# Chunk loads between the moves of x, ScalarE's output copies around a rounding, VectorE's extra work at the head of a slot

## What is computed

```python
w = np.exp(weight - np.max(weight, axis=-1, keepdims=True))
w = w / (np.sum(w, axis=-1, keepdims=True) + 1e-09)
x = np.einsum('hk,bskhg->bshg', w, x_unf)       # x_unf: each token and the 6 before it
h = x @ w_in                                     # first MLP
g = np.where(h >= 1, h, np.where(h <= -1, 0.0, (h + 1) ** 2 / 4))
x = g @ w_out
h = x @ w_in2                                    # second MLP
out = (h * (1.0 / (1.0 + np.exp(-1.702 * h)))) @ w_out2
```

## Time and profile before

| | |
|---|---|
| median of 3 runs | 1178.54 us (1177.29 to 1178.9) |
| the profiled execution | 1179.53 us |
| its span, first to last instruction | 1177.8 us |
| busy, share of the span | PE 97%, weight load 87%, DVE 70%, ACT 68%, POOL 36% |
| mean granted clock of PE | 0.993 of full speed |

### The profile page before, as it was taken

How to read it: one execution, slowest core, us unless ns; L and a number is a source line. 1 busy time by engine, 2 the same in 40 slices (tenths; PEclk the granted TensorE clock), 3 DMA queues, 4 the chain that set the end, 5 groups by cost and what they waited for, 6 DMA issues and landing times.

```text
span 1177.8 us, 25920 instructions
## 1 busy us (share of the span) xinstructions
PE 1146.4 (97%) x9382; PEld 1021.9 (87%) x9382; DVE 820.4 (70%) x1206; ACT 795.8 (68%) x1510; POOL 429.1 (36%) x425
## 2 busy tenths in 40 slices
PE   7999889999999999999999999999999999999998
PEld 4768679989989999889988999888988988899987
DVE  6877557677676867767677686767767676676633
ACT  4866476776867677686776767677676766765554
POOL 5892909053170714508062260804408062000000
PEclk9999989999999999999999999999999999999999
DMA  6312010001010010100001010010101000000001
GB/s 192 97 40 71 2 35 15 35 3 47 1 48 1 10 40 1 48 1 15 35 5 44 1 48 2 12 37 1 48 1 48 1 7 9 2 15 3 14 1 28
DMA packets 63857, 31.27 MB, mean 27 GB/s; under 512 B 56084, under 2 KB 60562, under 8 KB 63760
## 3 DMA queue, kind: packets, MB, share of 16 engines
q1 hardware_dynamic: 63760, 29.80, 9.5%
HBM read 23.09 MB, written 6.29 MB: 25 GB/s over the span
## 4 chain that ended last, share of the span: by engine, by line
PE 71%; ACT 11%; issue 6%; DVE 6%; POOL 5%; DVEq 0%; ACTq 0%; POOLq 0%
ACT raw L986 3%; ACT clip L936 3%; DVE gate L1103 3%; PE acc_all L748 3%; PE acc_all L762 2%; PE acc_all L754 2%; PE acc_all L757 2%; PE acc_all L759 2%; PE acc_all L765 2%; PE h_all L697 2%; PE h_all L699 2%; PE h_all L701 2%; PE h_all L692 2%; PE h_all L695 2%; PE acc_all L738 2%
## 5 line engine op out<-in xcount | busy, mean ns | idle before, releaser
L1109 DVE TENSOR_TENSOR g_lo<-gate,g_hi 128x512 fp32r<-128x512 f32 x232 | 190.0, 819 | 153.0 <-ACT g_hi L942 153.0
L942 ACT ACTIVATE g_hi<-gate 128x512 fp32r<-128x512 f32 x232 | 146.5, 632 | 201.0 <-DVE gate L1103 199.4
L1115 DVE TENSOR_TENSOR g_lo<-h_all,g_hi 128x512 fp32r<-128x512 f32 x256 | 175.0, 684 | 117.7 <-ACT h_all L953 115.8
L950 ACT ACTIVATE g_hi<-h_all 128x512 fp32r<-128x512 f32 x256 | 152.9, 597 | 87.1 <-PE h_all L703 58.1
L508 POOL TENSOR_TENSOR x_conv<-x_in,tap_w 128x384 f32<-128x384 f32 (+1 forms) x29 | 24.8, 875 | 508.8 <-ACT raw L986 506.5
L936 ACT ACTIVATE clip<-clip,half 128x512 f32<-128x512 f32 x256 | 184.3, 720 | 34.8 <-DVE clip L1094 32.6
L1094 DVE TENSOR_SCALAR clip<-h_all 128x512 f32<-128x512 f32 x256 | 174.8, 683 | 23.5 <-PE h_all L701 19.9
L508 POOL TENSOR_TENSOR prod<-x_in,tap_w 128x384 f32<-128x384 f32 (+1 forms) x174 | 181.2, 1065 | 4.2
L515 POOL TENSOR_TENSOR x_conv<-x_conv,prod 128x384 f32<-128x384 f32 (+1 forms) x174 | 179.8, 1055 | 1.6
L1103 DVE TENSOR_TENSOR gate<-h_all,clip 128x512 f32<-128x512 f32 x232 | 159.3, 687 | 19.5 <-ACT clip L936 8.7
L953 ACT ACTIVATE h_all<-h_all 128x512 f32<-128x512 f32 x256 | 151.6, 592 | 0.1
(11 more groups left out here) (281 smaller groups left out, 4766.0 us busy)
## 6 DMA issues: line engine op xcount, KB each, us to landing
x_in<-in_x SPq DMA_DIRECT2D x14, 960.0 KB, 4.8
out_y<-raw SPq DMA_DIRECT2D x360, 16.0 KB, 1.4
raw<-in_moe_w_out SPq DMA_DIRECT2D x6, 384.0 KB, 4.0
raw<-in_moe_w_in SPq DMA_DIRECT2D x4, 512.0 KB, 3.8
raw<-in_moe_w_in SPq DMA_DIRECT2D x8, 256.0 KB, 4.5
stage<-in_moe_w_out SPq DMA_DIRECT2D x2, 384.0 KB, 7.5
x_in<-in_x SPq DMA_DIRECT2D x1, 768.0 KB, 11.0
x_in<-in_x SPq DMA_DIRECT2D x2, 283.5 KB
```

The lines of the kernel that those rows point to most:

```text
L942: nc.scalar.activation(g1_hi[step.s % G_RING][:, :], gate1_of(step)[:, :], ACT.Copy).then_inc(g1_hi_ready, 1)
L950: nc.scalar.activation(g2_hi[step.s % G_RING][:, :], src, ACT.Gelu_apprx_sigmoid).then_inc(g2_hi_ready, 1)
L1109: nc.vector.tensor_tensor(g1_lo[k][:, :], gate1_of(step)[:, :], g1_hi[k][:, :].bitcast(FP32), ALU.subtract).then_inc(g1_lo_ready, 1)
L1115: nc.vector.tensor_tensor(g2_lo[k][:, :], bank2(step)[:, :], g2_hi[k][:, :].bitcast(FP32), ALU.subtract).then_inc(g2_lo_ready, 1)
```

## The change

The edit has four parts.

1. SP issues the moves of groups 0 to 2 (twelve transfers), then the loads of chunks 14 and 15, then the moves of groups 3 to 5. ACT rounds chunk 14 in slot 27 and chunk 15 in slot 28, not both in slot 31.
2. For tile 2's x the two parts are apart: transposes in slots 29 and 30 (both in 29 before), roundings in 29 and 30 (both in 29), low parts in 30 and 31 (both in 30).
3. ACT's copy of the main output sum stands ahead of the rounding of slot 8's gate, the copy of the rest behind it.
4. On DVE the additional work (transposes of x and of outputs, low parts of x, the last part of y) stands at the head of a slot, ahead of residue1, one slot later than before; the last part of y stays in slot 2.

```diff
-        EARLY = dict(move={3: [0], 4: [1], 5: [2], 6: [3], 7: [4], 9: [5]}, turn={7: [0], 10: [1]},
-                     hi={10: [0], 11: [1]}, lo={11: [0], 12: [1]})
-
-        LATE = dict(move={}, turn={13: [0, 1]}, hi={13: [0, 1]}, lo={14: [0, 1]})
+        EARLY = dict(move={3: [0], 4: [1], 5: [2], 6: [3], 7: [4], 9: [5]}, turn={8: [0], 11: [1]},
+                     hi={10: [0], 11: [1]}, lo={12: [0], 13: [1]})
+
+        LATE = dict(move={}, turn={13: [0], 14: [1]}, hi={13: [0], 14: [1]}, lo={14: [0], 15: [1]})
...
-            move_x()
+            sp.wait_ge(conv_step, 2 * CONV_STEPS)
+
+            sp.wait_ge(wp_ready, RAW_ORDER[0][-1] + 1 - DVE_CHUNKS)
+            move_x(range(MOVES // 2))
+
             for n in range(14, 2 * N_CHUNKS):
                 load_raw(n)
+            move_x(range(MOVES // 2, MOVES))
...
-                           24: [(13, 0)], 25: [(13, 1)], 31: [(14, 0), (14, 1), (15, 0), (15, 1)]}
+                           24: [(13, 0)], 25: [(13, 1)], 27: [(14, 0), (14, 1)], 28: [(15, 0), (15, 1)]}
...
+                if takes_out(tile) and s == OUT_SLOT:
+                    take_out(tile - 2, 0)
                 if one is not None:
                     round_gate1(one)
...
                 if takes_out(tile) and s == OUT_SLOT:
-                    take_out(tile - 2)
+                    take_out(tile - 2, 1)
...
                 solo = is_solo(tile, s)
+                at_y = s - shift_y(tile)
+                if takes_y(tile) and not solo and at_y == 2:
+                    take_y(tile - 1, 1 - side, 2)
+
+                if takes_out(tile) and s == OUT_SLOT + 6:
+                    turn_main(tile - 2)
+                if takes_out(tile) and s == OUT_SLOT + 7:
+                    turn_rest(tile - 2)
+                if prepares(tile):
+                    at = prep(tile)
+                    for part in at["turn"].get(s, ()):
+                        turn_x(tile + 1, part)
+                    for part in at["lo"].get(s, ()):
+                        split_x(tile + 1, 1 - side, part)
```

More of the change, by code:

```diff
@@ L431, in _, with move_x @@
             load(3)
-            def move_x():
-                sp.wait_ge(conv_step, 2 * CONV_STEPS)
-                sp.wait_ge(wp_ready, RAW_ORDER[0][-1] + 1 - DVE_CHUNKS)
-                for group in range(MOVES):
+            def move_x(groups):
+                for group in groups:
                     main = group < DM // BLOCK
@@ L965, in take_y, with take_out @@
                     nc.scalar.activation(rest[0:DR, :], y_part[0:DR, :], ACT.Copy).then_inc(y_from_act, 1)
-            def take_out(tile):
+            def take_out(tile, part):
                 main, rest = acc2
-                act.wait_ge(down2_done, (tile + 1) * F_TILES)
-                nc.scalar.activation(out_main, main[:, :], ACT.Copy).then_inc(out_copied, 1)
-                nc.scalar.activation(out_rest, rest[DR:P, :], ACT.Copy).then_inc(out_copied, 1)
+                if part == 0:
+                    act.wait_ge(down2_done, (tile + 1) * F_TILES)
+                    nc.scalar.activation(out_main, main[:, :], ACT.Copy).then_inc(out_copied, 1)
+                else:
+                    nc.scalar.activation(out_rest, rest[DR:P, :], ACT.Copy).then_inc(out_copied, 1)
             def take_x(tile, banks):
@@ L1202, in slot @@
                     residue1(before1)
-                at_y = s - shift_y(tile)
-                if takes_y(tile) and (at_y == 2 or solo and at_y == 1):
+                if takes_y(tile) and solo and at_y in (1, 2):
                     take_y(tile - 1, 1 - side, at_y)
-                if takes_out(tile) and s == OUT_SLOT + 5:
-                    turn_main(tile - 2)
-                if takes_out(tile) and s == OUT_SLOT + 6:
-                    turn_rest(tile - 2)
-                if prepares(tile):
-                    at = prep(tile)
-                    for part in at["turn"].get(s, ()):
-                        turn_x(tile + 1, part)
-                    for part in at["lo"].get(s, ()):
-                        split_x(tile + 1, 1 - side, part)
                 if two is not None:
```

## The result

The changed kernel takes **1175.97 us** (median, 1173.06 to 1176.88), beside 1178.78 us (1177.29 to 1179.02) for the kernel before on the same chip: a ratio of 0.9973, 95% interval 0.996 to 0.9986. It is faster, but by 0.3% where 1.0% was forecast, and it lies above the range. Its profiled execution took 1176.4 us, with a span of 1174.6 us.

The account below looks back on a forecast made before the run. PE, busy for 97% of the span, was taken as the bound, so only its standstills counted. 13.4 + 4.1 + 1.2 - 5.6 - 0.5 - 0.5 = 12.1 us gained, median 1178.54 to 1166.4 us; range 1159.5 to 1172.5.

Parts of the forecast that it names:

- the last part of y: Head of DVE's slot 2: PE loses 0.40 us in slot 3, 14 times, 5.6 us; 0.5 more in tile 2.
- the low parts of tile 2's x: Head of DVE's slots 30 and 31: wait for ACT's rounding delays g_lo once each, set at nothing, up to 0.8 us.
- the transposes of x: Head of DVE's slots 8 and 11: inputs ready slots before, so they cost next to nothing.
- The hole: PE's slots 37 and 38: ACT's wait for POOL, PE's standstill and the slow clock go, gaining 13.4 us.
- the queue of SP: Chunk loads between SP's moves: last twelve moves run from 98.8 to 106.8, last block in place at 108.6.
- the start of the convolution: POOL's convolution starts at 108.7, ends at 134.7; ACT comes to its move at 136.85, 2.1 us to spare.
- The wait for chunk 14: ACT's slot 27: the gate's rounding comes 1.7 us late; PE feels 0 to 1.0 us of it, taken as 0.5.
- Rival 4: Slots 12, 13: low parts of x meet POOL's additions, 1.0 us per tile, 13 us in all: 1180.6; chance 0.08.
- The port: DVE instructions with two SBUF inputs and POOL's exclude each other; trace agreed, price left to the fourth rival.
- The output copies: Slot 10 of a tile: main copy fits ahead of ACT's rounding, 0.34 us back 12 times, gaining 4.1 us.
- Slot 14: Slot 14 loses 0.20 us in twelve tiles; moving DVE's mid-slot work to the head regains half, 1.2 us.

Follow-up runs that it names:

- y_mid: Changed kernel with the last part of y again in the middle of DVE's slot 2, behind the clip: 1164.6 us, ratio 0.987.
- thin_add: Changed kernel with POOL's additions for tiles 3 to 15 cut to 8 columns, output not the reference's: 1171.75 us, ratio 0.9943.
- x_round_first: Changed kernel, y's last part and later tiles' low parts of x back mid-slot, ACT's roundings of tile 2's x ahead of the gate's: 1162.09 us.
- out_alone: Kernel before with only the two output copies on both sides of the rounding: 1173.25 us, ratio 0.9945.
- y_head_alone: Kernel before with only the last part of y moved to the head of DVE's slot 2: 1188.39 us, ratio 1.0098.
- turn_mid: Changed kernel with DVE's transposes of x for tiles 3 and later back in the middle of the slot before: 1173.03 us, ratio 0.995.
- thin_conv: Changed kernel with POOL convolving only the first of 8 heads for tiles 3 to 15, output not the reference's: 1168.08 us, ratio 0.9909.
- y_copy_first: Changed kernel with ACT's third copy of y ahead of the rounding of the gate in slot 1: 1165.16 us, ratio 0.989.
- short_pool: Changed kernel with POOL's convolution of tiles 4 to 15 in twice as many instructions of half the length: 1171.83 us, ratio 0.9939.
- short_best: x_round_first with POOL's convolution instructions of tiles 4 to 15 at half length: 1164.89 us, ratio 0.9883.

## Why the prediction was wrong

**What failed.** The profiled execution gained 9.0 us less than forecast (3.1 for 12.1). The step that failed is the price of the head of DVE's slot, which was too low. Its three wrong terms are the last part of y (priced at 0.40 us in each tile, measured 0.69, in tile 2 1.84 for the 0.9), the low parts of tile 2's x ("at nothing", measured 1.95 in slot 31), and the transposes of x ("costs next to nothing", 3.1 us in slot 12). Together they make 9.7 us. Slot 34 (slot 2 of tile 2), slot 13 and slot 14 add 1.8 us, and slot 10, chunk 14 and all others give 2.5 back.

**The hole, the queue of SP, the start of the convolution**: right, to a few tenths of a microsecond. The convolution itself ended at 136.08 and not at 134.7: it took 27.4 us, where 26.0 was called the most. ACT would have come at 136.85 by the forecast, so the room was 0.8 us and not 2.1; it was enough, and ACT came only at 140.68, since the slots before had grown.

**The last part of y** was the right mechanism with the wrong size; this is the largest miss (8.9 us against 5.2 in tiles 3 to 15, and in tile 2 slot 35 takes 6.17 us where y_mid has 4.33: 1.84 against 0.9). Three things were small each. The y part and g_lo are 0.72 us apart, and with that L742 is 0.57 us late, not 0.4 to 0.5. Then I took "a whole slot loses less (0.44) than the matmul is moved" over from slot 10; in slot 3 there is no such slack, the pairs of matmuls run 0.22 to 0.23 us apart with no gap up to the next slot. The slack of slot 10 has a cause that slot 3 lacks. Timeline of PE before, the partner of the late L748 in slot 10 of tile 4, and L748 in the undisturbed slot 3 of tile 5:

```profile
313.93 0.39 PE L745 MATMUL acc_all<-g_hi,w_down 64*128 64x512 f32 x1
...
353.89 0.39 PE L748 MATMUL acc_all<-g_hi,w_down 64*128 64x512 f32 x1
```

L748 was 314.50 - 312.34 = 2.16 us behind its slot's first matmul, where slot 3 has 1.59: 0.57 late, just as L742 is now. But L745 had already run alone, on time, so one pair fewer was left (by my estimate 0.57 + 0.10 - 0.23 = 0.44). Last, the first pair behind a wait takes 346.13 - 345.80 = 0.33 us, 0.1 more. That makes 0.57 + 0.1, about the 0.69 of the slot. The bound of 8.4 us for y was held out as the worst case; 0.69 in 14 tiles is 9.7. For tile 2 I added 0.5 us for one meeting with POOL; there are two in a row, the y part (1.16 us) and g_lo (1.37 us). Slot 34's 5.01 us are not y's, since y_mid has them too; they fall to 4.57 in thin_add, so they are the price of POOL's additions.

**The low part of tile 2's x at the head, "at nothing, up to 0.8"**, cost 1.95 us in slot 31. I had described the same wait as for y ("as y does below") and given it no price. x_round_first settles the cause: with ACT's rounding moved ahead, slot 31 takes 4.34 us. The wait for chunk 14, priced at 0.5 us, was the right mechanism and nearly the right size: ACT waited 1.65 us, and PE lost 0.38 of it, in slot 29. The kernels that round chunk 14 there have 4.41 to 5.19 us in slot 29; before, out_alone and y_head_alone have 4.33.

**Rival 4** named a mechanism of the right kind in the wrong place (and at 13 us, where it was 3.6 in slots 12 and 13). It expected the low parts of x to meet POOL's additions. Low parts at the head do take longer (up to 1.16 us in tiles 3 and later), but turn_mid (low parts at the head, no stall in slot 12) and x_round_first (low parts in the middle, stalls) exclude that PE pays for it there, and thin_add shows that the multiplications count too. It is the transpose, which needs nothing from POOL and which I had passed as free because "their inputs were ready slots before", that delays the next g_lo by 0.07 us into a race. I looked only at what an instruction waits for, not at whom it makes late. The rival's price had a slip as well: with the 1.2 us of slot 14 taken away, the sign turns at (12.1 - 1.2) / 13 = 0.84 us in each tile, not at 0.93.

**The port.** The Trainium skill, "SBUF — State Buffer", section "Who interferes with whom", says that a DVE instruction with two SBUF inputs and a GpSimd instruction that reads SBUF exclude each other and that issue order decides who blocks. Here g_lo took 1.45 us where the multiplication went first, and the multiplication took 1.33 us where g_lo did (turn_mid): the trace agrees, for multiplications as for additions. Which goes first can't be read from the recorded starts when these are 0.02 to 0.04 us apart.

**The output copies**: mechanism right, gain 5.5 instead of 4.1 us; the whole of slot 10's loss came back, also in out_alone. **Slot 14**: -0.5 instead of -1.2 us. thin_add and thin_conv show that its loss is POOL's (2.4 and 2.3 us go with the additions or the convolution), so that removing DVE's own work could give only a little.

## What to carry to other kernels

Work put at the head of an in-order engine's slot is free only if its input is older than what the engine would be waiting for anyway: look at where the *producer* stands in its own slot, and move the producer ahead as well (y_copy_first, x_round_first). Where PE has no slack in a slot, price a late operand at its whole lateness and, as here, 0.1 us more, not less. Look for the price in the slot that uses the late result, which can be two slots behind the wait (slot 29). An instruction that costs nothing can still shift its successor by a few hundredths of a microsecond into another engine's instruction; compare start times to those of the engine that shares the port.

## What was not expected of the hardware

- 0.07 us decide: a g_lo 0.10 us ahead of the start of a POOL multiplication kept its 0.69 us in all tiles, one 0.03 us ahead took 1.45 us in 20 of 66 (tiles 3 to 13 of six kernels).
- Halving POOL's instructions capped the long g_lo at 1.05 us in short_pool and 1.12 in short_best (up to 1.50 in the kernel after) and cost POOL time: a pair of additions of 128x384 without a wait takes 2.0 us, four of 128x192 about 2.3.
- The pair of matmuls behind a wait takes 0.33 us, others 0.22 to 0.23.
